# The last head pair of a pooled attention gets its own order of PSUM banks: sixteen of its eighteen score tiles go round all four pairs of banks

## The reference

```python
# q, k, v: (batch 4, heads 8, seq 1152, head_dim 64), f32
q_pool = q.reshape(B, H, S // 2, 2, D).mean(axis=3)          # 576 queries
scores = 1/sqrt(D) * np.matmul(q_pool, k.transpose(0, 1, 3, 2))
scores = scores - np.max(scores, axis=-1, keepdims=True)
attn = np.exp(scores)
attn = attn / (np.sum(attn, axis=-1, keepdims=True) + 1e-09)
out = np.matmul(attn, v)                                     # (4, 8, 576, 64)

x = out.transpose(0, 2, 1, 3).reshape(4, 576, 512)
xn = (x - mean) / sqrt(var + 1e-06) * g_ln
result = x + np.maximum(xn @ w_ch1, 0.0) @ w_ch2             # w_ch1 512x2048, w_ch2 2048x512
```

## Time and profile before

| | before |
|---|---|
| median of 3 runs | 808.1 us (807.71 to 808.26) |
| profiled execution, its time | 807.86 us |
| profiled execution, its span | 806.1 us |
| PE busy | 793.6 us (98%) |
| DVE busy | 643.1 us (80%) |
| ACT busy | 418.2 us (52%) |
| POOL busy | 445.2 us (55%) |
| granted clock of PE | 1.00 |

### The profile page before, as it was taken

The page is one execution under the profiler, slowest core; times in us unless marked ns, Lnnn a source line. Parts: engine busy times, 40 slices in busy tenths (PEclk is TensorE's granted clock), DMA queues, the critical chain, the costliest instruction groups (busy, mean ns, idle before and its releaser), DMA issues. The chain is left out here.

```text
span 806.1 us, 17053 instructions
## 1 busy us (share of the span) xinstructions
PE 793.6 (98%) x6472; PEld 663.7 (82%) x6472; DVE 643.1 (80%) x991; ACT 418.2 (52%) x941; POOL 445.2 (55%) x341
## 2 busy tenths in 40 slices
PE   8999999999999999999999999999999999999998
PEld 6777777787778777788779999989889989999897
DVE  6988889888889989888586767898867888766654
ACT  4676556576556665667723454543245454332431
POOL 3899989888888888787794222331411343131100
PEclk9999999999999999999999999999999999999999
DMA  8566534466444565321112211113322122422112
GB/s 187 135 146 147 136 92 99 114 147 146 117 89 102 133 147 136 73 71 40 32 53 62 95 54 53 66 53 126 96 66 59 59 81 65 148 76 63 57 40 79
DMA packets 39681, 75.36 MB, mean 93 GB/s; under 512 B 8880, under 2 KB 23472, under 8 KB 36016
## 3 DMA queue, kind: packets, MB, share of 16 engines
q1 hardware_dynamic: 38128, 73.88, 35.0%
q10 hardware_dynamic: 1472, 0.39, 0.3%
HBM read 69.54 MB, written 4.72 MB: 92 GB/s over the span
## 5 line engine op out<-in xcount | busy, mean ns | idle before, releaser
L588 POOL TENSOR_TENSOR acc<-acc,pT 128x576 f32<-128x576 f32 x160 | 239.4, 1496 | 23.2 <-ACT pT L932 0.4
L1299 PE MATMUL banks<-w2f,hT 128*128 128x512 f32 x864 | 214.3, 393 | 0.0
L932 ACT ACTIVATE pT<-banks 128x576 f32<-128x576 f32 x288 | 172.1, 652 | 38.3 <-PE banks L726 33.2
L1299 PEld LDWEIGHTS banks<-w2f,hT 128*128 128x128 f32 x864 | 160.3, 188 | 28.8 <-issue 0.2
L1043 DVE TENSOR_REDUCE pm<-banks 128x2 f32<-128x1024 f32 x128 | 153.4, 1222 | 34.6 <-PE banks L672 33.2
L728 PE MATMUL banks<-qT,kT 64*128 64x288 f32 x1728 | 162.4, 298 | 3.7 <-DVE pm L1043 2.6
L728 PEld LDWEIGHTS banks<-qT,kT 64*128 64x128 f32 x1728 | 133.7, 184 | 19.1 <-DVE pm L1043 8.0
L739 PE MATMUL banks<-pT,vn 128*64 128x288 f32 x1152 | 146.1, 408 | 0.0
L1377 ACT ACTIVATE hT<-mid 128x384 fp32r<-128x384 f32 x88 | 46.5, 528 | 182.1 <-DVE mid L1444 181.2
L398 POOL TENSOR_TENSOR w_sums<-w_stage 128x256 f32<-128x256 f32 x22 | 17.2, 783 | 212.2 <-DMA w_stage<-in_moe_w_ch_dram 206.4
L1444 DVE TENSOR_TENSOR mid<-banks,mid 128x384 f32<-128x384 f32 x154 | 85.5, 555 | 60.6 <-PE banks L1288 57.3
(11 more groups left out here) (122 smaller groups left out, 968.1 us busy)
## 6 DMA issues: line engine op xcount, KB each, us to landing
q_in_rows<-in_q_dram SPq DMA_DIRECT2D x56, 284.0 KB, 6.6
k_in_rows<-in_k_dram SPq DMA_DIRECT2D x56, 284.0 KB, 5.2
w_stage<-in_moe_w_ch_dram SPq DMA_DIRECT2D x24, 512.0 KB, 3.8
w_stage<-in_moe_w_ch_dram SPq DMA_DIRECT2D x48, 256.0 KB, 2.7
vn<-in_v_dram SPq DMA_DIRECT2D x16, 576.0 KB, 4.8
out_dram<-x SPq DMA_DIRECT2D x16, 256.0 KB, 3.2
q_in_rows<-in_q_dram SPq DMA_DIRECT2D x4, 256.0 KB, 3.0
k_in_rows<-in_k_dram SPq DMA_DIRECT2D x2, 288.0 KB, 4.0
```

Of the source, the lines that this page charges most:

```text
L588: nc.gpsimd.tensor_tensor(total, pT[:, h % 2, 0] if kt == 1 else total, pT[:, h % 2, kt], ALU.add).then_inc(chained, 1)
L932: nc.scalar.activation(pT[:, h % 2, kt], pair_banks("S", n)[:, :, 0:HW], ACT.Exp, scale=SCALE).then_inc(exp_done, 1)
L1299: last = nc.tensor.matmul(banks[:, k % 2 * (CT // 2) + kk], hT[:, k, a, tokens], w2f[:, (2 * u + k // 2) % 4, b], start=p == 0 and k < 2 a ...
```

## The change

One line is replaced. The last pair no longer takes the front part of `PAIR_STEPS`; its scores take the banks 6, 2, 4, 0 four times in turn and then 6 and 2. The tail has the same kinds of steps in the same order, with other banks: `O@4 E@1 Z@0` in place of `O@6 E@3 Z@5`; `PV@2 E@3 O@6 PV@0` stays.

```diff
-    PAIR_END = PAIR_STEPS[:PAIR_STEPS.index("O@6")] + "O@6 E@3 Z@5 PV@2 E@3 O@6 PV@0"
+    PAIR_END = 4 * "S@6 S@2 S@4 S@0 " + "S@6 S@2 O@4 E@1 Z@0 PV@2 E@3 O@6 PV@0"
```

## The result

| | before | after |
|---|---|---|
| median of 13 runs each | 807.63 us (806.99 to 808.38) | 806.57 us (805.31 to 807.62) |
| profiled execution, time and span | 807.86 us, 806.1 us | 805.31 us, 803.5 us |

The ratio is 0.9985, with a 95% interval of 0.9978 to 0.9992: 1.2 us less, between 0.6 and 1.8. The difference of the medians is 1.06 us. The forecast was 1.2 us less and a median of 806.9 us. The profiled execution after gained 2.55 us, more than the median, so its own parts have to be looked at.

What follows compares the result with a forecast made beforehand. PE was taken to bound the kernel. Removing 1.39 us of waits, less about 0.19 us waiting for POOL at `Z`, gives 1.2 us: 808.1 - 1.2 = 806.9 us, with an 8-in-10 range of 806.3 to 808.1.

Steps and rivals of the forecast that it cites:

- the three places: Last pair on PE: idle, released by an exponential, before score step 5, step 16 and first `O`; brackets 0.28, 0.29, 0.20 us.
- The removed waits: Last pair on PE: lost time at steps 5, 6, 16, 17 and `O` is regained, 1.39 us in sum.
- The term at `O`: First `O` of the last pair starts 0.50 us after the last score matmuls, against 0.22 in pair 14: 0.28 lost.
- The terms at the steps 5 and 16: Score waits of the last pair: 0.465 plus 0.095 us at steps 5 and 6, 0.445 plus 0.105 at 16 and 17.
- the first term: Wait at score step 5 with its follow-on at step 6: 0.465 + 0.095 = 0.56 us lost.
- the rival "not removed": Last pair's scores: a slower ACT, pitch over about 0.57 us, still holds PE at distance four; 807.8 us, chance 0.03.
- The moved waits: Waits of steps 2, 3, 9 and the tail's second `E`, `O` and `PV` change their source; all cost zero.
- The first rival: At `Z` of pair 15, POOL does not hold PE: 1.4 to 1.7 us gained, 806.6 us; chance 0.22.
- The wait at `Z`: At `Z` of pair 15, PE waits about 0.19 us for POOL's last addition, leaving a net gain of 1.2 us.
- The price of 0.5 us for one meeting more: Rival that POOL is later: one more collision with DVE costs 0.5 us, leaving 0.7 gained, 807.4 us; chance 0.10.
- the 3 us named as a sign of being wrong: Behind `Z`: prediction wrong if DVE's L417 still takes over 3 us and the fourth product waits.
- the rival's price, the whole gain: Rival at the fourth product: DVE's late L417 take the bank wait's place, no gain, 808.1 us; chance 0.10.

Runs made afterwards that it cites:

- e8: Kernel before with first `O` in banks 4 and 5, `Z` in bank 7, scores keeping their banks; one execution, 807.04 us, only its trace used.
- e1: Last pair's scores go round three pairs of banks (6 2 4 six times) in place of the changed kernel's four; 806.49 us, ratio 0.9983 to the kernel before.
- e7: Kernel before with other banks in score steps 3 to 7 alone, each taking banks used three or more steps ago; 807.07 us, ratio 0.9992.
- e3: Changed kernel with one of POOL's additions of the last half left out, so its sums lack a tile; 805.84 us, ratio 0.9979 to the kernel before.
- e6: Kernel before with one addition more on POOL in the last half, a tile counted twice; 807.74 us, ratio 1.0004.
- e5: Changed kernel with one addition more on POOL in the last half, a tile counted twice; 808.15 us, ratio 1.0008 to the kernel before.
- e4: Changed kernel with `Z` of pair 15 behind the third product in place of the second, and ACT's copy moved likewise; 806.14 us, ratio 0.9983 to kernel before.
- e9: Changed kernel with POOL's last tile of the last half added by DVE instead, sums complete; 805.88 us, ratio 0.9982 to the kernel before.

## Why the prediction was right, step by step

- **What bounds the kernel.** Right. PE set the pace, and the three places read from the earlier trace rows were the ones that lost time.
- **The removed waits, 1.39 us.** 1.49 measured at `O`. The term at `O` was 0.28; `O` now follows the last score by 401.14 - 400.52 = 0.62 where it was 0.91, so 0.29, and e8 has 0.27. The terms at the steps 5 and 16 were 0.56 and 0.55, 1.11 in all; measured are 1.20. The missing 0.09 is spread thin. Over the whole pair the cadence is now (400.52 - 392.04) / 16 = 0.53, where 0.535 was taken from a stretch in which five of eight scores return after three steps. These have no bracket, but e1 and e7 show that such a return costs a little. e7 shows the first term alone, 0.46, less 0.1 us because its steps return after three. The size of this term did not decide the gain: with 0.20 us less freed, e1 has its `Z` at the same place.
- **No score waits at distance four, and the last exponential is in time for `PV`.** Right. ACT's run ends at 402.20, `PV` starts at 403.05: 0.85 us of slack where 0.92 was expected. The working of the rival "not removed" has a slip: with its own starts and ends ACT's pitch would have to pass (401.72 - 0.05 - 0.65 - 393.42) / 13 = 0.585 us, not 0.57, to hold step 17; and no sum stands behind its 807.8.
- **The moved waits cost nothing.** Right; steps 2 and 3 have no bracket.
- **POOL's chain does not move and holds PE at `Z`.** Right. L336 starts 25.98 us after score step 0 before and 26.01 after. The first rival had DVE's additions meet POOL's at other moments. DVE did come to its first L989 0.45 us earlier, but it took 0.48 us longer there (1.44 us, against 0.96 in the earlier trace rows), and what follows starts at 7.36 us, where it was 7.34 before. That is why POOL's chain stayed as it was:

```profile
397.41 1.44 DVE L989 TENSOR_TENSOR acc_end<-pT 128x576 f32<-128x576 f32 x1 [4.23 <-ACT pT L932]
398.77 2.25 DVE L373 CAST xf<-xg_b 128x768 fp32r<-128x768 f32 x2
```

(Timeline of DVE after; before, this L373 starts at 399.86.)

The wait at `Z` was mis-sized: 0.19 expected, near the upper end of the 0.07 to 0.21 that its two hand-overs give, 1.48 - 1.16 = 0.32 measured. Of the 0.13, 0.09 is that PE came earlier, and the rest the hand-over, 417.60 - 417.46 = 0.14, the upper of the two values that stood there. e3 (the wait goes with one addition less) and e6 (it appears before, with one more) show the cause. The price of 0.5 us for one meeting more is too high: it sets 3.81 / 2 against the 1.42 of one row, but an addition more moves the end of the chain by 1.60 us (e5), so a meeting costs about 0.3 us. No run tests that rival.
- **Behind `Z` all stays earlier.** Right, and it was the step with the least margin. DVE's L1450 was expected 0.7 us ahead of the fourth product. It ends at 420.19, and the product starts about 2.1 us after 418.81, at 420.9. The two L417 took 3.37 us, which is over the 3 us named as a sign of being wrong, but the fourth product did not wait. What decides it is when DVE comes to the first L417. From the timelines of DVE and POOL, start to end in each trace's own time:

| | two L417 on DVE | first L336 on POOL | second L336 on POOL |
|---|---|---|---|
| changed | 416.34 to 419.71 | 417.42 to 419.44 | |
| e4 | 416.48 to 419.89 | 417.56 to 419.60 | |
| e7 | 418.20 to 420.59 | 418.27 to 420.31 | |
| e8 | 417.98 to 421.91 | 417.81 to 419.64 | 419.79 to 421.63 |
| before | 418.94 to 422.61 | 418.50 to 420.34 | 420.48 to 422.32 |
| e3 | 417.50 to 421.12 | 417.00 to 418.84 | 418.99 to 420.84 |
| e9 | 418.17 to 421.70 | 417.60 to 419.44 | 419.58 to 421.42 |

Where DVE comes first, the pair of L417 ends 0.27 to 0.29 us after POOL's first L336; where it comes behind POOL, 0.28 to 0.29 us after the second. That is the prediction's working (one L417 held to the end of the addition beside it, the other to the end of the next), and its 420.6 came at 419.71 + 1.11 = 420.82. So `h_lo` hangs on POOL's chain, which does not move with PE. In the kernel before, it is there 30.56 us after score step 0; in the changed kernel at 28.78, where the fourth product starts at 29.5. By this pattern, had DVE come to the first L417 behind the start of L336, 1.08 us later, `h_lo` would have been there at about 30.56 again and about 1.1 us of the gain lost. That is an estimate from these rows; it puts the rival's price, the whole gain, about right for this kernel. e8 lost all of its 0.28 us in this way, and e9, whose POOL chain ends earlier, 0.3.
- **The Trainium skill's rule** (Perfetto Trace Analysis, § Matmuls, different banks for independent groups) gave 1.39 us without POOL's chain. Its direction holds; e3, which shortens that chain, has 35.75 - 34.24 = 1.51.
- **The sum.** 1.2 us against 1.17 in the trace, 1.06 between the medians and 1.2 by the ratio. The median came 0.33 us below the 806.9 forecast, because the kernel before started 0.47 lower, at 807.63 in 13 runs and not the 808.1 of three, and the gain of the medians was 0.14 smaller. Two terms were mis-sized, the waits removed by 0.09 us and the wait on POOL by 0.13, and they all but cancel. That is the mechanism and not luck: what is freed beyond POOL's end is spent waiting for it, so only the 0.04 us of the hand-over counts. The chances had most on a change within 0.2%, and 0.15% came.

## What to carry to other kernels

A bank is free again after the time from the start of its matmuls to the end of the read; divide that by PE's step and round up, and that many bank pairs are enough (here 1.54 / 0.535, so three; two cost 3.7 us over 18 steps, and a fourth brought 0.2 us in the scores that nobody used). Before booking the gain, look for the next point where PE meets a chain that does not start from it, and compare the two arrival times: here 1.48 us freed met 1.32 us from POOL's end to PE's arrival, of which the hand-over takes 0.14, so 0.3 us of it was spent waiting. Beyond that point a gain can be lost in a step of its own: a few tenths of a microsecond in the start of L417 decide whether it ends behind POOL's first L336 or behind the second, 2 us later.

## What the runs showed of the hardware

- **The granted clock fell behind a single short idle stretch.** In e5 PE worked at a granted clock of 1.00 (2.4 GHz), was idle for 1.86 us, and right after it had 0.50 (1.2 GHz) for about 3 us, which cost 1.57 us, nearly as much as the wait itself. It did not come each time: by the mean clock, four of the ten executions had it. Idle stretches of 0.26 to 0.35 us on POOL (the changed kernel, e6) had no such effect; there the clock stayed at 1.00.
- **DVE's L417 is held over whole instructions of POOL.** Two of them take 2.39 us when the first starts 0.07 us before POOL's L336 (e7), 3.93 us when 0.17 us after (e8), 3.67 us when 0.44 us after (before), and 3.37 us when 1.08 us before it and so beside L592 (the changed kernel). The length follows from the table above: the pair ends 0.27 to 0.29 us behind the end of an L336, whenever it began. POOL's first L336 is longer too where DVE came first, 2.02 to 2.04 us against 1.83 to 1.84. The Trainium skill, VectorE: DVE Perf Modes, § Two Vector instructions with no wait between them, says that such an instruction reads one of its inputs through an interface shared with GpSimd; the order in which the two are served is read from these rows.
